# Attention stage: slot maximum in one reduction, constant column per head, and a moved pair of copies

## The reference

```
scores = q @ k_p.T / 8;  scores -= max(scores);  attn = exp(scores)
attn = attn / (sum(attn) + 1e-9);  x = attn @ v_p        # 4608 x 512 over all batches and heads
```

```
logits = x @ phi                                         # 4608 x 32
d = exp(logits - logits.max(0));  d /= d.sum(0) + 1e-9
slot_input = d.T @ x                                     # 32 x 512
```

## Time and profile before

| | |
|---|---|
| median of 3 runs | 499.55 us (496.21 to 501.06) |
| profiled execution, its time | 495.13 us |
| its span | 493.2 us |
| mean granted TensorE clock | 0.975 |
| PE / PEld busy | 441.1 / 354.8 us |
| DVE / ACT / POOL busy | 345.4 / 252.9 / 271.8 us |

### The profile page before, as it was taken

How to read it: one execution, slowest core, us unless ns; L and a number is a source line. 1 busy time by engine, 2 the same in 40 slices (tenths; PEclk the granted TensorE clock), 3 DMA queues, 4 the chain that set the end, 5 groups by cost and what they waited for, 6 DMA issues and landing times.

```text
span 493.2 us, 10576 instructions
## 1 busy us (share of the span) xinstructions
PE 441.1 (89%) x3781; PEld 354.8 (72%) x3781; DVE 345.4 (70%) x583; ACT 252.9 (51%) x553; POOL 271.8 (55%) x359
## 2 busy tenths in 40 slices
PE   1687898989899898589985999999999999999996
PEld 0676686878677686355654888788888888888885
DVE  6865889889898977374605899677777777777411
ACT  2346566665757565211223865556666555655410
POOL 0386776868677722023841533566667766666550
PEclk9988999999999999689998899999999999999999
DMA  8959597979869743989950015566666666666652
GB/s 249 294 138 285 215 271 258 304 203 297 198 259 267 265 167 111 314 296 387 396 211 1 1 44 98 114 143 147 144 131 133 134 134 133 133 133 132 128 122 48
DMA packets 125296, 91.74 MB, mean 186 GB/s; under 512 B 104776, under 2 KB 104784, under 8 KB 123216
## 3 DMA queue, kind: packets, MB, share of 16 engines
q1 hardware_dynamic: 125264, 91.32, 67.7%
HBM read 66.13 MB, written 9.44 MB: 153 GB/s over the span
## 4 chain that ended last, share of the span: by engine, by line
PE 64%; DVE 17%; DMA 7%; ACT 5%; issue 3%; SPq 2%; POOL 1%; DVEq 0%; ACTq 0%
PE banks L1375 12%; PE banks L1377 12%; PE banks L1376 12%; PE banks L1072 5%; DMA wslot<-in_moe_w 4%; PE banks L1352 3%; DVE attn L789 3%; PE banks L1171 3%; DVE smax L785 3%; PE banks L1104 2%; PE banks L1060 2%; SPq L423 2%; PE banks L1287 2%; PE banks L1124 2%; ACT kblk L566 2%
## 5 line engine op out<-in xcount | busy, mean ns | idle before, releaser
L1375 PE MATMUL banks<-wo_hi,uh 128*128 128x512 f32 x288 | 112.7, 391 | 0.0
L1377 PE MATMUL banks<-wo_hi,ul 128*128 128x512 f32 x288 | 112.1, 389 | 0.0
L1376 PE MATMUL banks<-wo_lo,uh 128*128 128x512 f32 x288 | 112.1, 389 | 0.0
L457 POOL TENSOR_TENSOR attn<-attn,srec 128x576 f32<-128x576 f32 (+1 forms) x40 | 45.9, 1146 | 73.4 <-DVE srec L803 73.4
L537 POOL TENSOR_TENSOR ul<-u_col,uh 128x1024 fp32r<-128x1024 f32 x30 | 72.2, 2406 | 25.6 <-ACT uh L566 25.6
L735 ACT ACTIVATE sq<-u,usum 128x1024 f32<-128x1024 f32 x36 | 41.5, 1152 | 41.7 <-DVE u L993 41.7
L1375 PEld LDWEIGHTS banks<-wo_hi,uh 128*128 128x128 f32 x288 | 54.2, 188 | 11.3 <-issue 0.3
L1376 PEld LDWEIGHTS banks<-wo_lo,uh 128*128 128x128 f32 x288 | 54.2, 188 | 11.1
L1377 PEld LDWEIGHTS banks<-wo_hi,ul 128*128 128x128 f32 x288 | 54.0, 188 | 11.3
L983 DVE TENSOR_REDUCE nmax<-banks 128x1 f32<-128x1024 f32 x36 | 43.6, 1221 | 23.4 <-PE banks L1352 23.4
L1072 PE MATMUL banks<-kblk,qT 128*128 128x144 f32 (+1 forms) x320 | 49.2, 299 | 6.9 <-ACT kblk L566 4.8
(11 more groups left out here) (160 smaller groups left out, 792.1 us busy)
## 6 DMA issues: line engine op xcount, KB each, us to landing
wslot<-in_moe_w SPq DMA_DIRECT2D x15, 2048.0 KB, 9.8
u_col<-u_blk SPq DMA_DIRECT2D x240, 64.0 KB, 2.1
qb<-in_q SPq DMA_DIRECT2D x32, 256.0 KB, 6.2
out<-osb SPq DMA_DIRECT2D x32, 256.0 KB, 2.5
kraw<-in_k SPq DMA_DIRECT2D x8, 640.0 KB, 6.9
vraw<-in_v SPq DMA_DIRECT2D x8, 640.0 KB, 5.4
kraw<-in_k SPq DMA_DIRECT2D x8, 512.0 KB, 5.9
vraw<-in_v SPq DMA_DIRECT2D x8, 512.0 KB, 4.0
```

The costliest lines, as they stand in the source:

```text
L457: pool.tensor_tensor(a, a, srec[bit(tile)][0:n, :].rearrange("p (j h) -> p j h", h=2)[:, :, :, None].to_broadcast([n, PAIRS, 2, SP]), ALU. ...
L1375: pe.matmul(ps[4 + par], uh[par][:, c, :], wo_hi[:, c, :], start=(c == 0), stop=False)
L1376: pe.matmul(ps[4 + par], uh[par][:, c, :], wo_lo[:, c, :], start=False, stop=False)
L1377: last = pe.matmul(ps[4 + par], ul[par][:, c, :], wo_hi[:, c, :], start=False, stop=(c == FC - 1))
```

## The change

1. `new_max`: PE writes the old maximum as one extra column next to the 128 columns that DVE reduces (four more matmuls in `lmax_t`, eight records, each one column), so a single reduction gives the new running maximum. The steps L839 (maximum with the old), L841 (difference) and L842 (diagonal) go. `mb_t` takes the maximum itself, repeated along the columns, as the stationary operand. `alpha_exp` computes exp(old - new) from the two buffers with scale -1 and the old one as bias.
2. Each head in `attn` gets a 73rd column that holds 1e-9 for good (HEAD = 73, PAIR = 147). `sums` adds 73 columns, and L799 with its wait goes. vpad has zeros at these columns. `exps`, `sub_max` and `norm` leave the column out. The last block of `aT_t` and `lt_t` has 76 columns and not 68, `dat_t` has 147 and not 145.
3. Order on ACT: `kT_evac` (t = 2, batches 1 to 6) and `vT_evac` (t = 4, batches 0 to 6) go from before `lt_evac` to after `exps`. `alpha_exp` goes from the head of t = 2 to its end. In the tail `d_exp` goes ahead of `alpha_exp`.
4. Three memsets of `attn` in place of four at the start.

```diff
-PAIR = 1 + 2 * SP
+HEAD = SP + 1
+PAIR = 1 + 2 * HEAD
...
+        def head_sums(n, par, t):
+            return attn[0:n, par, t, :].rearrange("p (j w) -> p j w", w=PAIR)[:, :, 1:].rearrange("p j (h c) -> p j h c", c=HEAD)
         def head_cols(n, par, t):
+            return head_sums(n, par, t)[:, :, :, 0:SP]
...
-                act.activation(alpha[par][:, :], mdiff[:, :], ACT.Exp).then_inc(sem("alpha"), 1)
+                act.activation(alpha[par][:, :], slot_max[par][:, :], ACT.Exp, scale=-1.0, bias=slot_max[1 - par][:, :]).then_inc(sem("alpha"), 1)
...
             def step(b, par, t, first, last):
                 tile = ahead(b, par, t)
-                if not first:
-                    if t == 2:
-                        alpha_exp(b - 1, 1 - par)
-                    if t == 5:
-                        datT_evac(b - 1)
+                if t == 5 and not first:
+                    datT_evac(b - 1)
                 if not (last and t + 3 >= TILES):
                     qT_evac(ahead(b, par, t + 3))
                 if t == 4 and not first:
                     dat_evac(b - 1)
-                if t == 2 and not first and not last:
-                    kT_evac(b + 1, 1 - par)
                 if t == 3 and not first:
                     v72_evac(b, par)
-                if t == 4 and not last:
-                    vT_evac(b + 1)
                 if not (first and t == 0):
                     lt_evac(ahead(b, par, t - 1))
                 if not (last and t + 2 >= TILES):
                     exps(ahead(b, par, t + 2))
+                if t == 2 and not first and not last:
+                    kT_evac(b + 1, 1 - par)
+                if t == 4 and not last:
+                    vT_evac(b + 1)
                 aT_evac(tile, 0)
                 if t == 2 and not first:
                     d_exp(b - 1)
                 aT_evac(tile, 1)
...
+                if t == 2 and not first:
+                    alpha_exp(b - 1, 1 - par)
...
-                dve.tensor_scalar(ssum1[par][0:n, :], ssum[par][0:n, :], TINY, None, ALU.add).then_inc(sem("ssum1"), 1)
-                dve.wait_ge(sem("ssum1"), g + 1)
...
-                dve.tensor_reduce(rowmax[:, :], b_tail[:, 0:P], AX.X, ALU.max).then_inc(sem("rowmax"), 1)
-                dve.wait_ge(sem("rowmax"), b + 1)
-                dve.tensor_tensor(new[:, :], rowmax[:, :], old[:, :], ALU.max).then_inc(sem("newmax"), 1)
-                dve.wait_ge(sem("newmax"), b + 1)
-                dve.tensor_tensor(mdiff[:, :], old[:, :], new[:, :], ALU.subtract)
-                dve.tensor_scalar(mdiag[:, :], ident[0:SLOTS, 0:SLOTS], new[0:SLOTS, :], None, ALU.mult).then_inc(sem("m_ready"), 1)
+                dve.tensor_reduce(slot_max[par][:, :], b_tail[:, 0:P + 1], AX.X, ALU.max).then_inc(sem("m_ready"), 1)
...
                 for j in range(PAIRS):
+                    pe.matmul(b_tail[32 * j:32 * (j + 1), 0:P], lmax[:, :], ident[:, :], start=True, stop=True, tile_position=(0, 32 * j))
+                for j in range(PAIRS):
+                    last = pe.matmul(b_tail[32 * j:32 * (j + 1), P:P + 1], ident[0:SLOTS, 0:SLOTS], slot_max[1 - par][0:SLOTS, :], start=True, stop=True,
+                                     tile_position=(0, 32 * j))
...
-                pe.matmul(b_tail[:, 0:SLOTS], ones[0:SLOTS, :], mdiag[:, :], start=True, stop=True).then_inc(sem("mb_ps"), 1)
+                pe.matmul(b_tail[:, 0:SLOTS], slot_max[par][0:SLOTS, :].to_broadcast([SLOTS, P]), ident[0:SLOTS, 0:SLOTS], start=True, stop=True).then_inc(sem("mb_ps"), 1)
```

More of the change, by code:

```diff
@@ L135, in build @@
         ssum = [bump(f"ssum{i}", [P, H]) for i in range(2)]
-        ssum1 = [bump(f"ssum1_{i}", [P, H]) for i in range(2)]
         srec = [bump(f"srec{i}", [P, H]) for i in range(2)]
         lmax = bump("lmax", [P, SLOTS])
-        rowmax = bump("rowmax", [P, 1])
-        mdiff = bump("mdiff", [P, 1])
-        mdiag = bump("mdiag", [SLOTS, SLOTS])
         alpha = [bump(f"alpha{i}", [P, 1]) for i in range(2)]
@@ L270, in steps @@
                 step(B - 1, 1, t, False, True)
+        def head_sums(n, par, t):
+            return attn[0:n, par, t, :].rearrange("p (j w) -> p j w", w=PAIR)[:, :, 1:].rearrange("p j (h c) -> p j h c", c=HEAD)
         def head_cols(n, par, t):
-            return attn[0:n, par, t, :].rearrange("p (j w) -> p j w", w=PAIR)[:, :, 1:].rearrange("p j (h c) -> p j h c", c=SP)
+            return head_sums(n, par, t)[:, :, :, 0:SP]
         def h_banks(par):
@@ L591, in vT_evac @@
             def vT_evac(b):
-                both_halves("vT", b, lambda hh: vpad[hh * D:(hh + 1) * D, :, V_LEFT + 1 + hh * SP:V_LEFT + 1 + (hh + 1) * SP], 1.0 / POOL)
+                both_halves("vT", b, lambda hh: vpad[hh * D:(hh + 1) * D, :, V_LEFT + 1 + hh * HEAD:V_LEFT + 1 + hh * HEAD + SP], 1.0 / POOL)
             def exps(tile):
-                a = attn[0:ROWS[tile[2]], tile[1], tile[2], :].rearrange("p (j w) -> p j w", w=PAIR)[:, :, 1:]
+                a = head_cols(ROWS[tile[2]], tile[1], tile[2])
                 act.wait_ge(sem("s_sub"), num(tile) + 1)
@@ L627, in dat_evac @@
                 act.wait_ge(sem("dat_ps"), dat_count(b, TILES - 1))
-                copy(dat[:, :], b_tail[:, 1:PAIR]).then_inc(sem("dat_sb"), 1)
+                copy(dat[:, :].rearrange("p (h c) -> p h c", c=SP), b_tail[:, 1:PAIR].rearrange("p (h c) -> p h c", c=HEAD)[:, :, 0:SP]).then_inc(sem("dat_sb"), 1)
             def datT_evac(b):
@@ L675, in _ @@
             lt_evac((B - 1, 1, 4))
+            d_exp(B - 1)
             alpha_exp(B - 1, 1)
-            d_exp(B - 1)
             dat_evac(B - 1)
@@ L764, in _ @@
             dve.memset(c_all[64:P, :, 4, :], NEG)
-            for j in range(PAIRS):
-                dve.memset(attn[:, :, :, j * PAIR:j * PAIR + 1], 1.0)
+            pair_cols = attn[:, :, :, :].rearrange("p a t (j w) -> p (a t j) w", w=PAIR)
+            dve.memset(pair_cols[:, :, 0], 1.0)
+            for hh in range(2):
+                dve.memset(pair_cols[:, :, 1 + hh * HEAD + SP], TINY)
             dve.memset(acc_slot[:, :], 0.0)
@@ L794, in sums @@
                 n, par, g = ROWS[tile[2]], bit(tile), num(tile)
-                a = head_cols(n, tile[1], tile[2])
+                a = head_sums(n, tile[1], tile[2])
                 dve.wait_ge(sem("s_exp"), g + 1)
@@ L798, in sums @@
                 dve.wait_ge(sem("ssum"), g + 1)
-                dve.tensor_scalar(ssum1[par][0:n, :], ssum[par][0:n, :], TINY, None, ALU.add).then_inc(sem("ssum1"), 1)
-                dve.wait_ge(sem("ssum1"), g + 1)
                 if not early:
                     dve.wait_ge(sem("attn_ready"), g - 1)
-                dve.reciprocal(srec[par][0:n, :], ssum1[par][0:n, :]).then_inc(sem("srec"), 1)
+                dve.reciprocal(srec[par][0:n, :], ssum[par][0:n, :]).then_inc(sem("srec"), 1)
             def batch_logits(b):
@@ L817, in vT_close @@
                 for hh in range(2):
-                    c = V_LEFT + 1 + hh * SP
+                    c = V_LEFT + 1 + hh * HEAD
                     last = dve.tensor_copy(vT[hh * D:(hh + 1) * D, :, :], vpad[hh * D:(hh + 1) * D, :, c:c + SP])
@@ L833, in new_max @@
             def new_max(b, par):
-                old, new = slot_max[1 - par], slot_max[par]
                 dve.wait_ge(sem("lmaxT_ps"), b + 1)
-                dve.tensor_reduce(rowmax[:, :], b_tail[:, 0:P], AX.X, ALU.max).then_inc(sem("rowmax"), 1)
-                dve.wait_ge(sem("rowmax"), b + 1)
-                dve.tensor_tensor(new[:, :], rowmax[:, :], old[:, :], ALU.max).then_inc(sem("newmax"), 1)
-                dve.wait_ge(sem("newmax"), b + 1)
-                dve.tensor_tensor(mdiff[:, :], old[:, :], new[:, :], ALU.subtract)
-                dve.tensor_scalar(mdiag[:, :], ident[0:SLOTS, 0:SLOTS], new[0:SLOTS, :], None, ALU.mult).then_inc(sem("m_ready"), 1)
+                dve.tensor_reduce(slot_max[par][:, :], b_tail[:, 0:P + 1], AX.X, ALU.max).then_inc(sem("m_ready"), 1)
             def d_sub(b):
@@ L1148, in l_t, with lmax_t @@
                 pe.matmul(b_lt[0:n, P:P + SLOTS], lt[bit(tile)][:, 0:n], fold4[:, :], start=True, stop=True).then_inc(sem("l_ps"), 1)
-            def lmax_t(b):
+            def lmax_t(b, par):
                 pe.wait_ge(sem("lmax"), b + 1)
@@ L1154, in lmax_t, with mb_t @@
                 for j in range(PAIRS):
-                    last = pe.matmul(b_tail[32 * j:32 * (j + 1), 0:P], lmax[:, :], ident[:, :], start=True, stop=True, tile_position=(0, 32 * j))
+                    pe.matmul(b_tail[32 * j:32 * (j + 1), 0:P], lmax[:, :], ident[:, :], start=True, stop=True, tile_position=(0, 32 * j))
+                for j in range(PAIRS):
+                    last = pe.matmul(b_tail[32 * j:32 * (j + 1), P:P + 1], ident[0:SLOTS, 0:SLOTS], slot_max[1 - par][0:SLOTS, :], start=True, stop=True,
+                                     tile_position=(0, 32 * j))
                 last.then_inc(sem("lmaxT_ps"), 1)
-            def mb_t(b):
+            def mb_t(b, par):
```

(10 more changed lines are left out.)

## The result

The changed kernel takes 540.59 us in the median, the kernel before 499.01 us in the same comparison. It is **slower by 8%**. The forecast was slower, at 522 us with a range of 505 to 533; the size lies outside.

The account below looks back on a forecast made before the run. PE was taken to pace the attention stage, DVE close behind. The profiled 495.13 us plus 15.3 gave 510.4, with the clock's 10 us 520.4; the median was expected about 2 us above, 522 us, range 505 to 533.

Parts of the forecast that it names:

- The wait for the key copies: PE before the vT transposes, t = 2, batches 1 to 6: one gap of about 2.0 us, net +0.16 us each.
- The wait for the value copies: PE before vphi (L1104), t = 4, batches 0 to 6: +2.29 us of pure wait, seven times.
- The two old gaps: PE's 0.86 us before L1161 (maximum) and 0.78 us before L1148 (logit copy) per batch; both should be gone.
- the sum: All terms over the profiled 495.13 us: +15.3 us without the clock, 510.4; +25.3 us with it, 520.4.
- the clock term: PE at half clock after some of the 13 new waits: seven falls taken, +10 us, bounds 0 and 18 us.
- rival 1: The clock holds through waits this short, all else as forecast: 510 to 515 us, chance 0.30.
- The steady worth of the constant column: L799 gone in the steady batches: 0, since DVE's slack hides its executions and PE still paces.
- The first batch: DVE paces until 37 us; L799's 1.37 + 0.75 us go: -2.1 us, between 0 and -2.1.
- The extra column: Four more matmuls, eight records, per batch on PE: +0.15 us, eight times; upper end 0.43 us, lower 0.
- Rival 3: Waits partly given back on PE by a less busy DVE: 0.9 us per batch, 505 us without clock falls, chance 0.06.
- Rivals 4 and 5: 4: copies end before PE arrives, 483 us, chance 0.06. 5: no change, 492 to 504 us, chance 0.06.

Follow-up runs that it names:

- filled kernel: The changed kernel plus needless matmuls on PE, seven ahead of each key-copy wait and eight ahead of each value-copy wait: 510.31 us, ratio 1.028.
- maximum only: The kernel before with only the one-reduction slot maximum, old order of copies and L799 kept: 494.93 us, ratio 0.994.
- column only: The kernel before with only the constant column (L799 gone), old slot maximum and old order of copies: 491.90 us, ratio 0.988.
- old order: The changed kernel with key and value copies back at their old places on ACT: 485.94 us, ratio 0.974.

## Why the prediction was wrong

**What held.** The wait for the key copies: 4.89 us from scores to vT transposes forecast, 5.04 measured (113.94 to 118.98), and about 2.0 us of wait against 2.12. The wait for the value copies: 5.04 us forecast from scores to vphi (133.56 to 138.60), 5.03 measured; L1097 waits 2.22 us in the row shown. They come six and seven times, as forecast. The two old gaps are gone. The filled kernel, which has these waits and hardly any half clock, is the forecast without the clock: span 507.8 us against 493.2, **+14.6 us**, where the sum had +15.3 and a batch of 24.8 us (25.0 measured). That it comes so close is in part luck: six batches are longer by 0.2 us each than forecast, and the first batch gained more, as told below.

**The step that failed** is the clock term: "I take seven, +10 us", with 18 us as its upper bound. All 13 waits brought half clock, and four times it ran on for twice the length, which the bound didn't allow for. A stretch costs more than the 1.4 us I worked out: two batches take 58.0 us, 50.0 with filled waits, for five stretches, so 1.6 us. 17 stretches at 1.6 us are 27 us. The medians of the changed and the filled kernel differ by 29.4 us, the spans by 27.1, the ends of the attention stage by 25.2 (247.96 and 222.80), for 17 stretches against one before the tail. With 27 for 10 the sum would have been 495.1 + 15.3 + 27 = 537.4 us; the profiled execution took 536.95. So close a match is luck again: the kernel before has two stretches of half clock in its first batch, 3.2 us at this price, which the changed kernel's profiled execution lacks and the sum doesn't take off, and the later stages took 286.9 us against 284.3.

I set the number of falls halfway between no fall and a fall each time, and rival 1 says that falls follow 3 us. The trace of the kernel before had a shorter gap that I passed over, in the first batch, and it was followed by a fall as the 3.14 us of the earlier trace rows were (the row of PE, then the busy time by stretch):

```profile
23.98 0.63 PE L1115 MATMUL banks<-ident,vT 128*72 128x128 f32 x4 [2.84 <-DVE vphi L825]
24.67:28.08 3.41, 3.41 (x18) 3.37 (x17) 1.22 (x5) 1.17 (x2) 2.77 (x3) 0.50 0.83 129
```

Both gaps of comparable length had brought a fall, so "each time" was the better reading of it.

The Trainium skill (TensorE: Matmul & The Clock Gate, section "Why this matters for your kernels") asks to avoid only PE gaps of more than about 3 us, and by that rule these would do nothing (rival 1). The runs don't bear it out: waits of 2.12 us brought half clock each time.

**Smaller misses, some of which cancel.** The steady worth of the constant column was put at 0. With the maximum only a batch takes 21.2 us, with both 20.5: 0.7 us per batch, since L799 inherits the wait for POOL's fold. In the changed kernel this is hidden behind the longer waits. The first batch gained about 4 us and not 2.1: the second batch's vT transposes stand at 57.3 us with the column only and at 57.0 with the old order, at 61.2 before. In the changed kernel the first value wait, its half clock and the first key wait consume it (61.0). The extra column was put at 0.15 us per batch; in order of time the eight one-column records stand 0.17 us ahead of the next group:

```profile
111.43 0.24 PE L1152 MATMUL banks<-slot_max,ident 32*32 32x1 f32 x8
111.60 0.55 PE L1073 MATMUL banks<-ident,kp 128*128 128x128 f32 x3
```

Rival 3 (waits given back elsewhere) did not occur: with the old order PE is busy 20.48 us per batch, before 20.50. Rivals 4 and 5 didn't either.

## What to carry to other kernels

Work that is moved behind an instruction which waits inherits that wait; ask first who waits for the moved work, and whether it ran ahead of need. When PE sets the pace, an idle gap costs more than its length: here 28.5 us of waits came with about 27 us of slower matmuls. Test the parts of a change apart: this one held a gain of 2.6% that its third part turned into a loss of 8%.

## What the runs showed that I had not expected

- Needless matmuls in a wait can pay: 15 per batch bring the changed kernel from 539.67 to 510.31 us, 5.4% less.
- After gaps of 1.3 us half clock follows only now and then (four of 13), so such a kernel's batches are uneven: 25.0 to 26.7 us in one execution.
- Half clock can come without a long gap: once behind gaps of 0.26 and 0.77 us (column only), once in a stretch where PE's list has no gap of 0.2 us (maximum only). Those batches took 1.8 and 1.4 us more than their neighbours. The cause is open.
- Removing one small DVE instruction that POOL holds up hands the hold-up to the next one: L842 at 0.84 us became L799 at 0.69 us.
